# VectorE's path over whole rows as a loop of seven heads and a last head, in a three-layer kernel on one core

## What is computed

```python
scores = scale * np.matmul(q, k.transpose(0, 1, 3, 2))
is_global = pos[None, :] < int(n_global)              # n_global = 8
is_local = (rel >= 0) & (rel < int(n_local))          # n_local = 96
scores = np.where(is_global | is_local, scores + bias[None], -1000000000.0)
a = np.exp(scores - np.max(scores, axis=-1, keepdims=True))
attn_out = np.matmul(a / (np.sum(a, axis=-1, keepdims=True) + 1e-09), v)
...
logits = np.einsum('bsd,de->bse', x, w_gate)          # and local_gate, from w_local
```

## Time and profile before

| | |
|---|---|
| median of 3 runs | 526.86 us |
| the profiled execution | 531.27 us, its span 529.4 us, 9448 instructions |
| mean granted TensorE clock | 0.981 of full speed |
| windows of the attention | from 15.8 us to about 105 us of the span |
| experts | from about 125 us to about 338 us |

### The profile page before, as it was taken

One profiled execution on the slowest core, in us unless ns is written; L12 is line 12 of the kernel. 1 busy time (PEld: TensorE's weight loads), 2 busy tenths in 40 slices (PEclk: granted clock), 3 DMA queues, 4 the chain that ended last, 5 costly groups with the idle time before them and its releaser, 6 DMA issues.

```text
span 529.4 us, 9448 instructions
## 1 busy us (share of the span) xinstructions
PE 502.2 (95%) x3416; PEld 438.2 (83%) x3416; DVE 270.1 (51%) x632; ACT 199.4 (38%) x425; POOL 108.6 (21%) x114
## 2 busy tenths in 40 slices
PE   9699999838999999999999899989999999999997
PEld 9488778738999999999899799978788878888885
DVE  4478787775114242414414411368887684454243
ACT  2798887403114141414414411436454333232010
POOL 3798862002112121212212111000000000000000
PEclk9899999957999999999999999999999999999999
DMA  8534426361943737464964600060000000000012
GB/s 333 211 120 133 182 79 250 123 238 47 384 158 133 303 141 290 155 273 178 386 281 174 271 24 20 22 221 0 1 1 1 1 1 20 21 20 21 20 60 80
DMA packets 19129, 71.16 MB, mean 134 GB/s; under 512 B 2702, under 2 KB 2702, under 8 KB 14864
## 3 DMA queue, kind: packets, MB, share of 16 engines
q1 hardware_dynamic: 16304, 63.88, 31.6%
q0 software_dynamic: 2640, 6.30, 3.4%
q10 hardware_dynamic: 144, 0.44, 0.2%
HBM read 62.49 MB, written 10.49 MB: 138 GB/s over the span
## 4 chain that ended last, share of the span: by engine, by line
PE 77%; DMA 8%; DVE 5%; issue 4%; ACT 3%; SPq 1%; POOLq 0%; DVEq 0%; POOL 0%; ACTq 0%
PE ps L1303 42%; PE ps L1332 19%; DMA w_sb<-in_w_experts 4%; PE ps L1235 3%; PE ps L1218 3%; PE ps L1198 3%; PE ps L1173 2%; PE ps L1158 2%; DMA x_rows<-x_tok 2%; ACT prob L645 2%; PE ps L1319 1%; PE ps L1404 1%; DMA x_tok<-y_rows 1%; DMA xin<-x_rows,token_at 1%; SPq L499 1%
## 5 line engine op out<-in xcount | busy, mean ns | idle before, releaser
L1332 PEld LDWEIGHTS ps<-xT,w_sb 128*128 128x128 f32 x1024 | 116.5, 192 | 4.2 <-issue 2.6
L1332 PE MATMUL ps<-xT,w_sb 128*128 128x128 f32 x1024 | 117.1, 275 | 2.2 <-DMA w_sb<-in_w_experts 1.8
L1038 DVE SCALAR_TENSOR_TENSOR hT_lo<-ps,hT_hi 128x512 fp32r<-128x512 f32 x32 | 22.1, 690 | 99.4 <-ACT hT_hi L699 99.2
L1047 DVE TENSOR_TENSOR w_lo<-w_sb,w_hi 128x1024 fp32r<-128x1024 f32 x32 | 37.0, 1219 | 39.7 <-ACT w_hi L710 39.7
L645 ACT ACTIVATE prob<-raw,row_min 128x256 f32<-128x256 f32 (+1 forms) x96 | 45.9, 480 | 15.1 <-DVE row_min L895 15.1
L1303 PE MATMUL ps<-w_hi,hT_hi 128*128 128x512 f32 x128 | 51.2, 400 | 0.0
L1303 PE MATMUL ps<-w_lo,hT_hi 128*128 128x512 f32 x128 | 49.9, 390 | 0.0
L1303 PE MATMUL ps<-w_hi,hT_lo 128*128 128x512 f32 x128 | 49.9, 390 | 0.0
L699 ACT ACTIVATE hT_hi<-ps 128x512 fp32r<-128x512 f32 x32 | 19.1, 596 | 75.5 <-PE ps L1332 75.5
L703 ACT COPY yout<-ps 128x512 f32<-128x512 f32 x16 | 9.4, 585 | 84.8 <-PE ps L1303 84.8
L895 DVE CUSTOM_DVE_ANT_0 raw<-ps,levels 128x256 f32<-128x256 f32 (+1 forms) x96 | 32.7, 394 | 7.6 <-issue 4.8
(11 more groups left out here) (173 smaller groups left out, 946.3 us busy)
## 6 DMA issues: line engine op xcount, KB each, us to landing
w_sb<-in_w_experts SPq DMA_DIRECT2D x32, 1024.0 KB, 9.2
v_sb<-in_vx SPq DMA_DIRECT2D x8, 640.0 KB, 4.1
q_raw<-in_q SPq DMA_DIRECT2D x8, 384.0 KB, 6.0
x_rows<-x_tok SPq DMA_DIRECT2D x2, 1536.0 KB, 7.9
x_tok<-y_rows SPq DMA_DIRECT2D x12, 256.0 KB, 5.9
out_x<-o_sb SPq DMA_DIRECT2D x12, 256.0 KB, 2.0
k_raw<-in_kx SPq DMA_DIRECT2D x7, 432.0 KB, 4.8
wtr<-in_w_tok_rT SPq DMA_DIRECT2D x6, 384.0 KB
```

What stands on the lines that cost most here:

```text
L1038: dve.scalar_tensor_tensor(hT_lo[:, part, :], ps[:, 1 + half, :].rearrange("p (c q) -> p c q", c=4), 0.0, hT_hi[:, part, :].bitcast(F32), ...
L1047: dve.tensor_tensor(quarter(w_lo, par, q), quarter(w_sb, par, q), w2_hi_quarter(q).bitcast(F32), ALU.subtract).then_inc(s_w2_lo, 1)
L1332: last = pe.matmul(ps[:, 1 + half, f * P:(f + 1) * P], w_sb[:, par, c // 2, j:j + P], xT[:, c, :], start=(c == 0), stop=(c == DC - 1))
```

## The change

VectorE's 48 written-out tiles of the whole rows become an engine loop over heads 0 to 6 and, written out behind it, head 7. For that the helpers take the half, the bank and the columns as arguments, the row sums of the whole rows are kept in one place for all heads, `lg` is zeroed at the start so that every head adds to it (in the windows too), and the waits count one more on s_sum. In the loop some waits are left out, and a new semaphore, s_seen, is signalled by an instruction that carries the wait for the scores. The windows keep their order.

```diff
@@ -232,6 +232,7 @@
         s_den = sem("den")
         s_x_done = sem("x_done")
         s_sum = sem("sum")
+        s_seen = sem("seen")
         s_part = sem("part")
         s_exact = sem("exact")
         s_in_tile = sem("in_tile")
@@ -643,7 +644,7 @@
                 of = raw[:, g % 4, b * WINDOW:b * WINDOW + w] if w < S else raw_rows[:, b, :]
                 m = 2 * (g % 4) + b if w < S else b
                 act.activation(where, of, ACT.Exp, bias=row_min[:, m:m + 1], scale=-1.0,
-                               accum_out=den[:, h % 2, i, b:b + 1]).then_inc(s_exped, 1)
+                               accum_out=den[:, h % 2 if w < S else 0, i, b:b + 1]).then_inc(s_exped, 1)
 
             def windows():
                 def turned(g):
@@ -792,6 +793,7 @@
             dve.memset(tiny, 1e-9)
             dve.memset(tiny_s[:], 1e-9)
             dve.memset(neg_big[:], -BIG)
+            dve.memset(lg[:], 0.0).then_inc(s_sum, 1)
             dve.wait_ge(s_table_in, 16)
             then(dve.tensor_copy(nloc_f[:], con("numbers").bitcast(I32)))
 
@@ -827,52 +829,48 @@
                 wait(dve, s_back, q - 1)
                 dve.tensor_copy(outT[:, 1, :], ps[:, 6, 0:GROUP * P]).then_inc(s_ot1, 1)
 
-            def shares(q):
-                h, half = q // 2, q % 2
-                tiles = slice(GROUP * half, GROUP * half + GROUP)
+            def shares(q, half, home, constant):
                 dve.wait_ge(s_exped, 2 * GROUP * (q + 1))
-                sums = den[:, h % 2, tiles, :].rearrange("p i b -> p (i b)")
-                if q < LAST - 1:
-                    dve.wait_ge(s_back, q + 1)
-                dve.tensor_tensor(den_e[:, half, :], sums, tiny if q < LAST - 1 else tiny_s[:], ALU.add).then_inc(s_rank, 1)
+                sums = den[:, home, GROUP * half:GROUP * half + GROUP, :].rearrange("p i b -> p (i b)")
+                dve.tensor_tensor(den_e[:, half, :], sums, constant, ALU.add).then_inc(s_rank, 1)
                 dve.wait_ge(s_rank, q + 1)
                 dve.reciprocal(rec[:, half, :], den_e[:, half, :]).then_inc(s_den, 1)
 
-            def share_and_back(q):
-                return (rec[:, q % 2, :].rearrange("p (i b o) -> p i b o", i=GROUP, o=1),
-                        ps[:, back_bank(q), 0:GROUP * TURNED].rearrange("p (i c) -> p i c", i=GROUP))
-
-            def logits(q):
-                share, turned_back = share_and_back(q)
+            def share_and_back(half, bank):
+                return (rec[:, half, :].rearrange("p (i b o) -> p i b o", i=GROUP, o=1),
+                        ps[:, bank, 0:GROUP * TURNED].rearrange("p (i c) -> p i c", i=GROUP))
+
+            def logits(q, half, bank):
+                share, turned_back = share_and_back(half, bank)
                 dve.wait_ge(s_back, q + 1)
                 dve.wait_ge(s_den, q + 1)
-                dve.tensor_tensor(part[:, q % 2, :].rearrange("p (i b e) -> p i b e", i=GROUP, b=B),
+                dve.tensor_tensor(part[:, half, :].rearrange("p (i b e) -> p i b e", i=GROUP, b=B),
                                   turned_back[:, :, P:].rearrange("p i (b e) -> p i b e", b=B),
                                   share.to_broadcast([P, GROUP, B, E + 1]), ALU.mult).then_inc(s_part, 1)
 
-            def rows_of_x(q):
-                share, turned_back = share_and_back(q)
-                h, tiles = q // 2, slice(GROUP * (q % 2), GROUP * (q % 2) + GROUP)
-                dve.tensor_tensor(x_tok.rearrange("p (b i) d -> p i b d", b=B)[:, tiles, :, h * DH:(h + 1) * DH],
+            def rows_of_x(half, bank, columns):
+                share, turned_back = share_and_back(half, bank)
+                tiles = slice(GROUP * half, GROUP * half + GROUP)
+                dve.tensor_tensor(x_tok.rearrange("p (b i) d -> p i b d", b=B)[:, tiles, :, columns],
                                   turned_back[:, :, 0:P].rearrange("p i (b d) -> p i b d", b=B),
                                   share.to_broadcast([P, GROUP, B, DH]), ALU.mult).then_inc(s_x_done, 1)
 
-            def add_logits(q):
-                h, half = q // 2, q % 2
+            def add_logits(q, half):
                 to = lg.rearrange("p (b i) e -> p i b e", b=B)[:, GROUP * half:GROUP * half + GROUP]
                 of = part[:, half, :].rearrange("p (i b e) -> p i b e", i=GROUP, b=B)
                 dve.wait_ge(s_part, q + 1)
-                if h == 0:
-                    dve.tensor_copy(to, of).then_inc(s_sum, 1)
-                else:
-                    dve.wait_ge(s_sum, q - 1)
-                    dve.tensor_tensor(to, to, of, ALU.add).then_inc(s_sum, 1)
+                dve.wait_ge(s_sum, q + 1)
+                dve.tensor_tensor(to, to, of, ALU.add).then_inc(s_sum, 1)
 
             def normalise(q):
-                shares(q)
-                logits(q)
+                h, half = q // 2, q % 2
                 if q < LAST - 1:
-                    rows_of_x(q)
+                    dve.wait_ge(s_back, q + 1)
+                shares(q, half, h % 2, tiny if q < LAST - 1 else tiny_s[:])
+                logits(q, half, back_bank(q))
+                if q < LAST - 1:
+                    rows_of_x(half, back_bank(q), slice(h * DH, (h + 1) * DH))
+                add_logits(q, half)
 
             def windows():
                 def turned(g):
@@ -909,33 +907,44 @@
                         turned(2 * r)
                     for q in turned_back_at(r):
                         normalise(q)
-                        add_logits(q)
 
             def whole_rows():
                 dve.wait_ge(s_rest_in, 16)
                 distances(far[:, 0:REL], far[:, REL:], 0, dist, range(QT), s_ch_all, s_mask_all)
-                for g in range(PAIRS):
-                    h, i = g // QT, g % QT
-                    if i == 0 and h:
-                        dve.wait_ge(s_raw, 2 * g)
-                        then(dve.tensor_scalar(dist[:], dist[:], SLOPE_RATIO, None, ALU.mult), s_ch_all)
-                    dve.wait_ge(s_scores, g + 1)
-                    for b in range(B):
-                        wait(dve, s_exped, 2 * (g - 1) + b + 1)
-                        dve.tensor_tensor_reduce(raw_rows[:, b, :].rearrange("p (c k) -> p c k", c=2),
-                                                 ps[:, 2 * b:2 * b + 2, 0:HALF],
-                                                 dist[:, i, :].rearrange("p (c k) -> p c k", c=2), -DH ** -0.5, 3.0e38,
-                                                 ALU.add, ALU.min, row_min[:, b:b + 1]).then_inc(s_raw, 1)
-                    for b in range(B):
-                        dve.wait_ge(s_pt0, 2 * g + b + 1)
-                        wait(dve, s_av, g)
-                        dve.tensor_copy(probT_rows[:, b, :].rearrange("p (c k) -> p c k", c=2),
-                                        ps[:, 4:6, 0:HALF]).then_inc(s_cp0, 1)
-                    if g % QT == 2 * GROUP - 1:
-                        second_half(g // GROUP)
-                    if i % GROUP == GROUP - 1:
-                        normalise(g // GROUP)
-                        add_logits(g // GROUP)
+
+                def rows_of_head(h, last):
+
+
+                    for i in range(QT):
+                        dve.wait_ge(s_scores, QT * h + i + 1)
+                        dve.sem_inc(s_seen, 1)
+                        for b in range(B):
+                            dve.tensor_tensor_reduce(raw_rows[:, b, :].rearrange("p (c k) -> p c k", c=2),
+                                                     ps[:, 2 * b:2 * b + 2, 0:HALF],
+                                                     dist[:, i, :].rearrange("p (c k) -> p c k", c=2), -DH ** -0.5, 3.0e38,
+                                                     ALU.add, ALU.min, row_min[:, b:b + 1]).then_inc(s_raw, 1)
+                        for b in range(B):
+                            dve.wait_ge(s_pt0, 2 * QT * h + 2 * i + b + 1)
+                            dve.tensor_copy(probT_rows[:, b, :].rearrange("p (c k) -> p c k", c=2),
+                                            ps[:, 4:6, 0:HALF]).then_inc(s_cp0, 1)
+                        if i == QT - 1:
+                            dve.wait_ge(s_av, QT * h + QT)
+                            dve.tensor_copy(outT[:, 1, :], ps[:, 6, 0:GROUP * P]).then_inc(s_ot1, 1)
+                        if i % GROUP == GROUP - 1:
+                            half = i // GROUP
+                            q, bank = 2 * h + half, back_bank(LAST) if last and half else 7
+                            shares(q, half, 0, tiny_s[:])
+                            logits(q, half, bank)
+                            if not last:
+                                rows_of_x(half, bank, bass.ds(DH * h, DH))
+                            add_logits(q, half)
+
+                with dve.Fori(0, H - 1) as h:
+                    rows_of_head(h, False)
+                    dve.wait_ge(s_raw, 2 * QT * h + 2 * QT)
+                    dve.tensor_scalar(dist[:], dist[:], SLOPE_RATIO, None, ALU.mult).then_inc(s_ch_all, 1)
```

(8 more changed lines are left out.)

## The result

The kernel after takes **524.61 us** (median; 523.48 to 527.77), the kernel before, run beside it, 527.66 (526.34 to 529.40): ratio 0.9942, 95% interval 0.993 to 0.9955, or 3.0 us less (2.4 to 3.7). Measured once more on another chip it was 0.9943 [0.9922, 0.9963]. The prediction said 523.1, in a range of 521.6 to 527.0, and faster.

What follows compares the result with a forecast made beforehand. It took VectorE's 3.50 us "issue" gap, a far jump's code fetch behind data, as the bound. From the median 526.86, 3.4 for the wait and 0.4 for the clock dip gave 523.1 us, range 521.6 to 527.0 (forecast's own 521.6 to 524.7).

Steps and rivals of the forecast that it cites:

- What bounds the kernel: Before VectorE's first reduction: 3.50 us of "issue", its code fetch after the far jump standing behind 2.35 MB of data.
- the loop itself, the zeroing, the waits: Whole-rows loop never issued, `lg` memset covered by the table wait, waits on s_sum and others reordered: 0 each.
- Head 0's two copies become additions: In VectorE's windows: additions of 0.20 us each replace copies, in time VectorE has spare: 0.
- The distance of the jump: VectorE's skip at the start falls from about 583 instructions to 152 to 158; all 3.50 us won, or nothing.
- Blocks that end near 60 and near 185: VectorE's code: first block ends near instruction 60, second near 185, both held at the start; windows start at 177 to 183.
- half a win: Rival at the windows' start: only tile 0 fits, tile 1 reduces at 15.8; 526.2 us, chance 0.08.
- Held already: The windows' start lies in the second block's last instructions, so the jump needs no fetch; chance 0.69.
- a forward jump always fetches: One ground for the missed-entry rival: VectorE starts at 15.8 again, 526.9 us; missed entry has chance 0.17.
- The third tile's block arrives at 15.8: Tile 2 needs the next block, arriving about 15.8; ScalarE gets its minimum at 16.2, k_lo moves by 3.5 us.
- The half-clock dip goes: TensorE's half clock from 24 to 25 us may go with the first hole filled: 0 to 0.75, half taken, 0.4.
- The sum: In the first 26 us: -3.4 for the wait and -0.4 for the dip make -3.8, subtracted from the median 526.86.
- The slower rival: A block's end falls inside the odd experts' tile loop and each of 8 tiles fetches: 530.3 us, chance 0.06.

Runs made afterwards that it cites:

- the written-out form: Kernel after with its loop replaced by seven heads written out, 471 instructions skipped: 529.28 us, ratio 1.0028; again 528.78, 1.0015.
- both kernels with the windows first: Kernel after with VectorE's windows ahead of the whole rows: 527.67 us, ratio 0.9986; the same with 24 cheap instructions run ahead: 525.15, 0.9953.
- the 24 instructions: Kernel after with windows first, plus 24 cheap instructions run in the wait for the table (branch 471, target 620): 525.15 us, ratio 0.9953.
- with 15 and with 20 more instructions: Kernel after plus never-run instructions in the skipped whole rows: 15 (windows start at 189) 528.37 us, ratio 1.0005; 20 (194) 527.52, 0.9998.
- 10 more instructions: Kernel after plus 10 never-run instructions in the skipped whole rows, windows starting at 184: 524.6 us, ratio 0.995.
- `far` late: Kernel before with the 1088 KB table `far`, unused in the windows, sent for at 11.6 us instead of 4.6: 526.72 us, ratio 0.9968.

## Why the prediction was right, point by point

- **What bounds the kernel; the loop itself, the zeroing, the waits: nothing.** Right: the written-out form has them all and gains nothing.
- **Head 0's two copies become additions, 0.** Wrong: it cost 0.6 us in the profile after and 1.2 in the second one. The price of 0.20 us came from one row of an addition with GpSimd idle. In the profile of before, four of the 14 additions, all beside GpSimd's k_lo, take 0.65 us; no copy takes over 0.20, whatever GpSimd does. And VectorE had no time to spare there, since the next head's first reduction stood right behind.
- **The distance of the jump, 152 to 158 instructions skipped and a start at 177 to 183.** 149 and 174; the direction held and the count was 3 to 9 too high (and before has 584 for "about 583").
- **Blocks that end near 60 and near 185.** 192 is shown. Ends at 448, 576 and 704, in steps of 128, fit both kernels with the windows first and the loops; 64 is worked out from those steps. I had taken the step as 103 to 124 from packets against busy instructions. The margin was 18 instructions and not 2 to 8, which is why the first two tiles (8 instructions) and all of "half a win" were safe. That the entry lay inside was luck in part: the rows gave steps of 103 to 124, the prediction took 125, and at 103 the second block would have ended at 163, short of every start that it counted.
- **Held already.** Right: going forward, the block being run and the next are held. The rival "a forward jump always fetches" fell with the kernel after and with the 24 instructions.
- **The Trainium skill** ("Runtime: NRT & Kernel Launch", Instruction fetch mechanics) states that a taken branch out of the current window of two blocks waits for a DMA. These runs agree, with 2.69 against 0.42 us. Its size of 256 instructions a block doesn't hold here. With it the windows would have stayed in reach with 15 and with 20 more instructions, and those lost the gain.
- **The third tile's block arrives at 15.8.** Wrong twice, without a cost. Tiles take four instructions each, so tile 2 is 182 to 185 in the kernel after and lies ahead of the edge; it reduced at 15.02, when TensorE had its scores. And the packet ran at 13.08; with the 2.0 us from a packet to its first instruction, its code was there at about 15.1. Only with 10 more instructions did this block hold tile 2 up, by 0.2 us. The rest followed: ScalarE's next exponential, forecast for 16.2, was at 16.09, k_lo 3.24 us earlier (3.5).
- **The half-clock dip goes, 0.4.** It went (0.94 to 1.00) and gave 0.9, the lead growing from 3.24 to 4.1 us. Why it went is not shown. None of the seven profiles whose first two tiles waited for no code has it, and five of the other seven do. But it is there with `far` late, where TensorE stood for only 0.35 us before tile 2 (half clock at 21 and 22 us), and of the written-out form's two profiles, with holes of 1.58 and 1.59 us, only the second has it. So it doesn't follow from the first hole alone. The shift didn't stay either: the additions took 0.6 of it.
- **The sum, 3.8 us; measured 3.0.** In the pair of profiles it is 3.24 for the wait, 0.9 for the dip and -0.6 for the additions, 3.5 in all, where the prediction had 3.4, 0.4 and 0. That the last two nearly cancel is luck. The rest of the miss is the size of the wait, which was read from a single profile. In five profiles with a missed jump the first reduction began at 15.77, 15.14, 14.99, 15.04 and 14.85, and before's was the latest. In four with the jump held and the whole rows first it began at 12.53, 12.37, 12.78 and 11.60, when the scores were there. The means differ by 2.8 us (15.16 less 12.32). ScalarE's lead over the profile of before near the attention's end, which has the dip and the additions in it, is 3.55 in the mean of the four and 0.38 in that of the five: 3.2 us, close to the 3.0. (The 12.27 of the chain is the end of the second tile's scores; the first tile's, all that the first reduction needs, ended at 11.84. From there the wait was 3.9 us in before, 3.0 to 3.3 in the other four, and 0.04 or 0.05 where the jump was held.) The profiled execution of before was 4.4 us above the median, and I had put all of that elsewhere. The other 0.8 us of the miss in the absolute time is the base: 526.86 in three runs, 527.66 in twenty.
- **The slower rival.** Fell: an edge inside the loop over pairs and inside the tile loop cost nothing measurable.

## What to carry to other kernels

A path that isn't taken costs time where the jump over it leaves the code that the engine holds, and then the fetch also waits for data queued ahead of it; an "issue" gap right behind a branch, with one instruction packet in it, is the sign. Count from the branch to the target and to the ends of the blocks: put the likely path first where a jump at its end is covered, shorten or loop the unlikely one, or move a load that nobody needs yet from ahead of the fetch. Such a gain is fragile, since 15 instructions more in the skipped body undid this one, and it should be sized from several profiles. And what is rewritten for the path that isn't taken should leave the other as it is: two copies turned into additions cost 0.6 to 1.2 us here.

## What the runs showed of the hardware

- From the start of the instruction packet to the first instruction behind it there were 2.0 to 2.1 us in every missed case at the start (13.69 to 15.77, 13.11 to 15.14, 13.49 to 15.45, 11.92 to 13.96), and 2.0 and 1.8 with the DMA engines nearly idle (101.50 to 103.53, 102.64 to 104.48).
- What varies is the time from the branch to the packet: 1.0 us with idle queues (100.5 to 101.5), 3.8 to 4.5 us behind data (9.2 to 13.7 in before), 2.9 us with `far` out of the way. A missed jump takes about 3 us from the branch at best, and 5.8 to 6.6 at the start of this kernel, of which 3.0 to 3.9 were not covered by the wait for the scores.
- VectorE's jumps back over the edge at 704, in two nested loops, sent for nothing and waited for nothing (two packets of q14 from 125 to 330 us, and 99.3 us of waits for ScalarE, as without an edge there). The jumps forward to beyond the next block waited each time, for 2.7 to 4.8 us of "issue", or until 13.96 with `far` late.
- An addition of 128x54 on VectorE took 0.20 us alone, 0.65 beside GpSimd's k_lo and up to 1.76 beside its q_lo, and beside q_lo it ended within 0.1 us of q_lo's end (33.11 and 33.03, 32.81 and 32.73, 35.71 and 35.63). A copy of the same size took 0.20 us beside either. What the two engines share there, the traces don't show.
- The first tile's scores end anywhere from 11.5 to 12.7 us in the fourteen profiles of nearly the same code, so one pair of profiles says little on the first microsecond.
